# Attention on one Trainium2 core: products with v made for two steps together, and q requested ahead of v

## What is computed

```python
def _attn_ref(q, k, v):                 # (4, 8, 576, 64) each
    scores = scale * np.matmul(q, k.transpose(0, 1, 3, 2))
    rel = pos[:, None] - pos[None, :]
    mask = (rel >= 0) & (rel < 64)
    scores = np.where(mask, scores, -1000000000.0)
    scores = scores - np.max(scores, axis=-1, keepdims=True)
    attn = np.exp(scores)
    attn = attn / (np.sum(attn, axis=-1, keepdims=True) + 1e-09)
    return np.matmul(attn, v)
...
```

## Time and profile before

| What | us |
|---|---|
| Median of three runs | 1027.08 (1026.12 to 1031.17) |
| The profiled execution's own time | 1028.99 |
| Its span, first to last instruction | 1027.3 |
| TensorE busy in the span | 983.7 |
| ScalarE busy in the span | 442.3 |
| Mean granted TensorE clock | 0.986 of full speed |

### The profile page before, as it was taken

One profiled execution on the slowest core, in us unless ns is written; L12 is line 12 of the kernel. 1 busy time (PEld: TensorE's weight loads), 2 busy tenths in 40 slices (PEclk: granted clock), 3 DMA queues, 4 the chain that ended last, 5 costly groups with the idle time before them and its releaser, 6 DMA issues.

```text
span 1027.3 us, 19801 instructions
## 1 busy us (share of the span) xinstructions
PE 983.7 (96%) x5424; PEld 845.0 (82%) x5425; DVE 553.9 (54%) x1324; ACT 442.3 (43%) x1088; POOL 480.1 (47%) x560
## 2 busy tenths in 40 slices
PE   7999899999999999999999969999999999999994
PEld 6889799798998998989988758887878888887773
DVE  5667422425234234242246867766777777767672
ACT  6898633334333342342244333343434434434441
POOL 4666477756777788778635311212121121122121
PEclk9999899999999999999999989999999999999997
DMA  8999477959999999999425923978495959668111
GB/s 184 212 220 220 101 227 254 296 188 327 309 310 336 308 307 323 312 298 296 131 82 175 295 81 107 274 248 265 140 270 142 288 166 263 191 219 252 52 55 49
DMA packets 257486, 225.23 MB, mean 219 GB/s; under 512 B 84620, under 2 KB 189068, under 8 KB 257424
## 3 DMA queue, kind: packets, MB, share of 16 engines
q1 hardware_dynamic: 219344, 185.02, 60.9%
q0 software_dynamic: 9280, 28.62, 8.1%
q10 hardware_dynamic: 28800, 10.83, 4.7%
HBM read 140.68 MB, written 85.82 MB: 220 GB/s over the span
## 4 chain that ended last, share of the span: by engine, by line
PE 69%; DMA 7%; DVE 6%; issue 6%; ACT 5%; ACTq 3%; DVEq 1%; SPq 1%; POOL 1%; POOLq 0%
PE bank L1467 20%; PE bank L1484 19%; PE bank L1569 11%; PE bank L1561 10%; DMA part<-out,yrow 4%; ACT hq L903 3%; PE bank L1399 2%; DMA out<-y_sb,yrow 2%; ACTq L886 2%; DMA q_raw<-q 2%; PE bank L1421 1%; ACT he L912 1%; PE bank L1383 1%; PE bank L1509 1%; PE bank L1407 1%
## 5 line engine op out<-in xcount | busy, mean ns | idle before, releaser
L1569 PE MATMUL bank<-W,he 128*128 (+1 forms) x960 | 229.0, 394 | 8.1 <-DVE he L1204 7.7
L1561 PE MATMUL bank<-W,xe 128*128 (+1 forms) x960 | 227.9, 393 | 8.8 <-DVE xe L1174 8.8
L1569 PEld LDWEIGHTS bank<-W,he 128*128 128x128 f32 x960 | 179.0, 188 | 52.7 <-issue 13.3
L1561 PEld LDWEIGHTS bank<-W,xe 128*128 128x128 f32 x960 | 182.0, 190 | 48.0 <-issue 9.2
L1484 PE MATMUL bank<-W,gs 128*128 128x512 f32 x864 | 217.2, 395 | 0.0
L1467 PE MATMUL bank<-xs,W 128*128 128x384 f32 x832 | 203.9, 343 | 3.4 <-DVE xs L1081 1.7
L1484 PEld LDWEIGHTS bank<-W,gs 128*128 128x128 f32 x864 | 160.6, 188 | 30.9 <-DVE gs L1086 0.7
L744 POOL DMA_INDIRECT out<-y_sb,yrow x40 | 40.7, 1018 | 288.1 <-DVE y_sb L1212 281.3
L903 ACT ACTIVATE hq<-bank 32x256 f32<-32x256 f32 x320 | 119.8, 374 | 108.4 <-issue 99.3
L1467 PEld LDWEIGHTS bank<-xs,W 128*128 128x128 f32 x832 | 151.4, 191 | 11.1 <-issue 3.1
L644 POOL TENSOR_TENSOR raw<-raw,xT 128x512 fp32r<-128x512 f32 x112 | 145.2, 1296 | 9.0
(11 more groups left out here) (176 smaller groups left out, 1001.7 us busy)
## 6 DMA issues: line engine op xcount, KB each, us to landing
W<-split_weights SPq DMA_DIRECT2D x112, 512.0 KB
raw<-moe_w SPq DMA_DIRECT2D x128, 256.0 KB
split_weights<-xT SPq DMA_DIRECT2D x112, 256.0 KB, 4.0
split_weights<-raw SPq DMA_DIRECT2D x112, 256.0 KB
xg<-x_by_expert ACTq DMA_DIRECT2D x160, 64.0 KB
v_pairs<-v SPq DMA_DIRECT2D x16, 544.0 KB, 4.2
q_raw<-q SPq DMA_DIRECT2D x16, 288.0 KB, 3.7
out<-zeros SPq DMA_DIRECT2D x12, 384.0 KB
```

Source lines behind the costliest of these rows:

```text
L1561: ins = nc.tensor.matmul(h2_ps[par][:, f * 512:(f + 1) * 512], xe[par][:, xl, d * P:(d + 1) * P], weights(e, wl, d * FE + f * 512), start= ...
L1569: ins = nc.tensor.matmul(ye_ps[par][:], he[par][:, hl, c * P:(c + 1) * P], weights(e, wl, W1COLS + c * DM), start=(c == 0 and wl + hl == 0 ...
```

## The change

In `unit_loads` the request for q of unit u + 2 goes ahead of that for v of unit u. On TensorE the products with v leave their place behind the scores of each step. In every second step (m = 0, 2, 4) both `attend(n - 5)` and `attend(n - 4)` stand between `turn_p(n - 3)` and the mask and scores; in the odd steps there are none. The end of the attention, after body 7, is rearranged in the same way. No instruction is added or removed, and no wait is changed in itself. The lists of the other engines stay as they are.

```diff
                 u = i * 2 + par
-                load_v(u, par)
                 if not last:
                     load_q(u + 2)
+                load_v(u, par)
                 if not (last and par):
                     load_w(i + par, 1 - par)
...
                     if not (first and m < 3):
                         turn_p(n - 3, (m - 3) % 6)
+                    if m % 2 == 0:
+                        for back in (5, 4):
+                            if not (first and m < back):
+                                attend(n - back, i if m >= back else i - 1, (m - back) % 6)
                     score_waits(n, i * 2 + m // 3, m % 3)
                     score(m // 3, m % 3)
-                    if not (first and m < 4):
-                        attend(n - 4, i if m >= 4 else i - 1, (m - 4) % 6)
                     if more and m % 3 < 2:
...
             turn_p(last - 3, 3)
-            attend(last - 4, LOOP - 1, 2)
+            for m in (1, 2):
+                attend(last - 6 + m, LOOP - 1, m)
             turn_p(last - 2, 4)
             attend(last - 3, LOOP - 1, 3)
             turn_p(last - 1, 5)
-            attend(last - 2, LOOP - 1, 4)
-            attend(last - 1, LOOP - 1, 5)
+            for m in (4, 5):
+                attend(last - 6 + m, LOOP - 1, m)
```

## The result

The changed kernel takes 1041.39 us, the median of four runs (1038.89 to 1043.96); the kernel before, run beside it, 1028.76 (four runs). The ratio is 1.0123 (1.0090 to 1.0156), so the change costs some 12.6 us. The ratios here are worked out from all executions of a kernel and can differ by up to 0.2% from the quotient of two medians. The direction was forecast, the size was not: 1033.2 is 8.2 us short, and 1041.4 lies above the range's 1038.5. Of the 8.2, 1.7 are the kernel before, which read 1028.76 here and not 1027.08; the change itself cost 12.6 where 6.1 was forecast.

A forecast was written before the change was run, and what follows sets the result against it. TensorE was taken to set the pace, 12.83 us a pass. Start +1.1, six passes +5.9, waits gone -1.96, end +1.0: together +6.1, so 1033.2 against the median 1027.08; 8 in 10 for 1025.0 to 1038.5.

The forecast's parts named there:

- Part 1, merging: Products with v on TensorE: three change-overs fewer in a pass, 3 x 0.29 = 0.87 us, TensorE's own need falling to 11.96.
- the rival in which nothing is merged: Second block of a pair pays its 0.29 again: a pass of 14.7, +11 us, 1038.5; chance 0.03.
- Part 2, moving: Attention passes: products ahead of even steps' scores bring waits of 1.85 us, a pass of 13.82, 0.99 longer than 12.83.
- the three chains: TensorE waits once hidden behind odd steps' products: ScalarE's q copy 0.97, GpSimd's norm 0.32 twice, VectorE's result copy 0.19.
- A: Start of a step's six score matmuls on TensorE; a number behind it names the step.
- Part 3, q ahead of v: Load requests: the 1.96 us of waits in six passes go; v, w and k come later, k costing 0.2 at the start.
- The margin of 0.9 for k: Odd units' last k lands 7.1 after step 4's scores start and is wanted at 8.0: hidden, by 0.9.
- Start and end: Attention before and after the six passes: start +0.9, with k +1.1; end +1.0.
- A5: Start of step 5's scores at the kernel's start, forecast at 19.69 us.
- A6: Start of step 6's scores, forecast at 22.40 for 21.49, after the second block waits until 21.69.
- The clock: Rival: TensorE's clock falls to half in the attention too, costing 3.5 us, 1036.7; chance 0.05.
- TensorE keeps the pace: Rival: none of the waits come, seven passes give 7 x 0.87 and the 1.96 goes: -8.1, 1019.0; chance 0.10.

## Why the prediction was half right

**What bounds the kernel before:** right as far as it went. Where TensorE waits for nothing, it sets the pace at 12.83; only the last of the six passes was so, the others took 12.87 to 13.56. Not seen was how near the next bounds stand: the loads (the shortest passes are 12.88 to 12.99, with the DMA share at 1.08, in the runs above) and, with less to load, whatever gives 12.82 in the kernel with merged products.

**Part 1, merging:** right. Two blocks in one stream took 0.87, forecast 0.85. The rule that the forecast weighed there, from the Trainium skill ("TensorEngine Tiling (Array Packing)", Key Properties), that a change of mode drains TensorE, fits this: the second block changes no mode and pays nothing. It did not decide the result, for what the drain gave back was less than what the waits took. This rules out the rival in which nothing is merged.

**Part 2, moving:** the three chains, their number and their order were right, and the middle stretch to 0.03. The step that failed is the length of the handovers in the other two: they were read in the earlier trace rows, in body 7, and used for the loop. In the stretch from step 0 to 2, ScalarE's copy of q was put at 0.87 + 1.77 + 0.87 = 3.51 behind the scores; in the loop it ends at 3.72 (the maximum 0.09 later, the copy another 0.14 behind it). That alone gives the 5.50 of the run with VectorE's copy halved: +0.20. VectorE's copy of q is no term of the sum at all. In body 7 it ends 0.7 ahead of ScalarE's and may be left out; in the loop it ends at A + 3.50, all six k transposes wait for it and hold TensorE for 0.55 behind it, and that adds the other 0.07 (5.57). In the stretch from step 4 to 0 the copy of the result was put 0.75 behind the maximum; it is 1.01: +0.24 (4.38 to 4.62). With 0.03 of the middle stretch it makes 0.54 a pass, 3.2 over six. The written-out kernel has both terms as forecast and passes of 13.87 to 14.01, and body 7 of the changed kernel has a first stretch of 5.27; so the place of reading, not the mechanism, was at fault. What in the loop makes the handovers longer stays open.

**Part 3, q ahead of v:** right that the waits for q go, and that v, w and k behind it are hidden in passes this long. Not right as "1.96 us that the change gives": the kernel before with q first shows that the 2 us of the queue only move on to k, and the kernel with v first and merged products behind the scores shows that q first is needed. The margin of 0.9 for k was worked out for a long pass; in a pass of 13 it is gone.

**Start and end:** +1.96 for +1.1. A5 comes at 20.79, forecast 19.69 and 0.2 for k. Part of the miss is not of the change: step 2's mask stands at 14.15 instead of 13.76, since step 1's six scores, at 11.91, lasted 1.49 instead of 0.95. The granted clock reads 1.00 in both traces there, but 1.49 is what six scores take in the stretches at half clock (44.67 in the run with both copies of q halved). The order of before with other loads or written out has that mask at 13.72 to 14.23, so this differs from execution to execution. The rest is waits of 0.33 for v (at 17.85), 0.21 for k (at 19.56) and 0.3 for the copy of the result, of which v's had no price. From A5 on it went as forecast: 2.66 to A6, forecast 2.71. The end cost +0.75 for +1.0.

**The sum:** attention +10.2 in the trace, forecast +6.1: 3.2 from the loop's terms, 0.9 from the start, 0.3 from the three passes that took 14.45 or 14.46 instead of 14.36, less 0.25 at the end: 4.15, the whole difference. The median moved by 12.6 (9.3 to 16 by the interval), 2.4 more than the trace's attention. No experiment separated this, and the traces leave it open: from the next layer's first matmul to the end all kernels run the same code, and it took 901.5 to 912.0 us in the eighteen traces, 908.8 in that of before and 908.3 in that of after. The clock there differs too (half for 7 us right behind the attention in the profile of before, at no place from 105 to 160 us in that of after).

**The rivals.** The clock did not fall in the attention in the changed kernel's trace, whose longest wait there is 1.1 a pass; it did in four others, told of in the last section. The Trainium skill ("TensorE: Matmul & The Clock Gate", Why this matters for your kernels) warns of idle gaps between bursts, and each of these falls came in or behind a wait; but a wait of 2.77 was followed by none, so the length of one wait does not decide it here. "TensorE keeps the pace", at 1019, would have failed for a reason that the forecast did not name: with the products behind the scores and less to load, passes still took 12.82, and with all loads 12.88 and more. No kernel of the study is shown to beat the kernel before; the nearest, merged behind the odd steps' scores with v's small request moved, takes the same time within its interval.

## What to carry to other kernels

Read the length of a handover in the same code form as the one you price: the same copy can end 0.2 to 0.7 us later behind the scores in a loop than in a body written out, and this shows only once the chain is laid bare. Before taking matmuls out from between two groups, list every chain that they covered and follow both engines that share a copy, not the one that looks later. And when an engine's work shrinks by some per cent, ask which engine or queue is next: here merging took 7% off TensorE's work by the forecast's prices, and no pass came out more than 0.02 us shorter.

## What the runs showed of the hardware

- The request that follows v's large load (544 KB) in SyncE's queue is the slow one, whichever load it is: v's small one (2.24 at 41.87, 1.2 to 3.2 in the looped kernels), q (1.39 at 64.73 in the kernel before with v's small request moved, 0.7 to 1.4), or w (2.14 at 53.33, 1.2 to 2.7). In the kernel before, where neither stands right behind v's large one, q takes 0.33 and w 0.39.
- In a loop, VectorE's copy of the result starts behind idle time of up to 0.43 that waits for no semaphore ("issue"), the first maximum of a pass starts 0.09 later than written out, and ScalarE's copy of q ends 0.23 later. In undisturbed passes of the kernel before, all of it is hidden.
- The clock fell to half in the attention of four kernels, for 3.4 to 6.9 us each time: in the one with 12.2 us of waits for q three times, in a wait of 2.76 (from 38.8) and behind waits of 2.16 and 1.99 (over 30 to 100 us it was granted at 0.93); in the written-out changed kernel once, at 57.7, behind a wait of 1.95; with both copies of q halved once, at 43.6, behind waits of 1.24 and 0.43 for k; in the changed kernel with v's small request moved once, at 19.3, in a wait of 2.08. Waits of 2.77 in the kernel before with q ahead of v (ended at 35.72) and of 2.02 in the first of these four (ended at 56.78) were followed by no fall, and the changed kernel, with no wait over 1.1 in its passes, kept the full clock in its trace.
